# Attention scores over 64 of TensorE's 128 rows: even row tiles in the lower half, odd ones in the upper

## The chip, the cores and the metric

The kernel runs on one core of one Trainium2 chip. The metric is device time in microseconds (us) of one execution. Besides TensorE (PE in the profile; its weight loads are PEld) the core has VectorE (DVE), ScalarE (ACT), GpSimd (POOL) and the DMA queues issued from SyncE (SP) and POOL. They run side by side and meet at semaphores.

## The reference

Attention over 4 batches and 8 heads of 768 positions and 64 numbers each, with a window of 96 positions back and 8 global positions, and then two mixtures of experts over the 3072 rows:

```python
def _attn_ref(q, k, v, n_global, n_local):
    scores = scale * np.matmul(q, k.transpose(0, 1, 3, 2))
    keep = is_global | is_local                 # j < 8, or 0 <= i - j < 96
    scores = scores + bias[None, :, :, :]       # -slope[h] * distance
    scores = np.where(keep, scores, -1000000000.0)
    a = softmax(scores)
    return np.matmul(a, v)

def reference(**kwargs):
    x = _attn_ref(...)                          # to rows of 512
    x = _moe_ref(x=x, ...)                      # 8 experts, 512 -> 1024 -> 512
    return _moe2_ref(x=x, ...)                  # the same with a bias by modality
```

## The kernel before

A setup block builds constants, starts the first loads and works out on DVE whether the window fits the banded form (`banded`). In the banded form `banded_attention` runs; `general_attention` is compiled beside it and not executed with these inputs. After attention come routing and the two mixtures (`stages`), which the change leaves alone but for the tiles in which the second gate's weights wait.

Attention is cut into **slots**, one for each head of each batch (32, and two to run out). All engines go through the same slots in the order written out in their function `slot`. In slot h, TensorE does, in this order:

- `score(h, 0)` and `score(h, 1)`. A score takes one row tile of 128 queries against 256 keys (row tile 0: 128 keys) into one of three PSUM banks, `t.ps_s[:, n % 3]`. It waits until DVE has taken the score three before.
- one unit of `transpose_qk` for the next pair of heads (three 128x128 transposes into half 0 or 1 of `t.ps_qk`), then `weigh_v` on row tiles 2 to 5 of head h-2 (16 matmuls of 65 columns)
- `transpose_p(h-1, 0)`, `score` 2 and 3, the next unit of `transpose_qk`, `transpose_p(h-1, 1)`, `weigh_v` on row tiles 0 and 1 of head h-1
- in even slots `logits` (6 x 2 matmuls of 8 columns), then `score` 4 and 5, and `transpose_p(h-1, 2)`; in odd slots `transpose_x` before and after it, for the pair of heads finished last.

Every f32 matmul is two instructions in the trace, so a pair of scores is "x4".

A pair of heads has four units: units 0 and 1 are turned in the even slot and carry q, units 2 and 3 in the odd slot and carry k. A unit of q holds three row tiles of both heads: after the transpose head 2p lies in partitions 0 to 63 and head 2p+1 in 64 to 127. ACT's `move_qk` copies it to `t.qT` with two instructions of 64 partitions each (lines 512 and 513), one for each head. In `t.qT` each head has all 128 partitions, the half that is not its own being zero (lines 138 and 139 write these zeros once). So the matmul contracts over 128 rows, and the keys of the other head are multiplied by zero. The keys are copied with all partitions at once: the 8 global keys (line 517) and three blocks of 128 (line 519).

On ACT the unit moved in a slot stands behind exponentials 1 and 3 of that slot, and `move_x` (line 527), two copies of the finished pair's transpose, behind the sixth in odd slots. TensorE waits for `qk_moved` before the first score of an even slot and before each unit of `transpose_x`; it waits for `xT_moved` before it turns units 0 and 1.

DVE takes each score (`bias`, line 425), copies the turned probabilities (`move_pT`, line 434), and `finish`es a head (lines 440 to 446).

POOL stores zeros to the padding rows of `x2` (called mixed in the trace) out of the zero half of `t.qT` (line 198) and loads and splits the first expert's weights through the ring `t.stage`, all beside attention.

Of the kernel before, what the change touches and what calls it, by code (L numbers as in the profile page):

```python
# [12 lines left out]
P = 128  # L13
B, H, S, DH = 4, 8, 768, 64
NQ = S // P
# [62 lines left out]
def setup_block(nc, t, s, q, k, v, n_global, n_local, w_gate, w_gate2, mod_bias):  # L78

    with nc.Block() as block:  # L80
# [45 lines left out]
        def _(dve):  # L126
# [11 lines left out]
            dve.memset(t.qT[DH:P, 0, :, :], 0.0)  # L138
            dve.memset(t.qT[0:DH, 1, :, :], 0.0)

# [18 lines left out]
def banded_attention(t, s, q, k, v, x1, x2, w1, w2, modality_id):  # L159

    NS = H * NQ
    QKU = 4 * H // 2
# [28 lines left out]
    def gpsimd(pool):  # L191

        pool.dma_start(t.modi[:, :, :], modality_id.bitcast(I32)
                       .rearrange("(i p w) -> p i w", p=P, w=2)).then_inc(s.modality_loaded, 16)
        pool.wait_ge(s.rows_loaded, 1)

        for j in range(NT + 1, MAXT + 1):
            pool.dma_start(x2[j * P:(j + 1) * P, :].rearrange("(p r) n -> p (r n)", r=2),
                           t.qT[DH:P, 0, :, :].rearrange("p j n -> p (j n)")[:, 0:2 * D])\
                .then_inc(s.x2_cleared, 16)  # L200
# [15 lines left out]
        pool.wait_ge(s.x2_cleared, 16 * (MAXT - NT))  # L216

    def sync(sp):
        flag = sp.value_load(t.banded[0:1, 0:1], min_val=0, max_val=1)
        with sp.If_eq(sp.to_reg(flag), 1):  # L220
            def load(b, p):

                sp.wait_ge(s.qk_turned, QKU * b - QKU + 4 * p + 4)
# [29 lines left out]
    def tensor(pe):  # L253
        flag = pe.value_load(t.banded[0:1, 0:1], min_val=0, max_val=1)
        with pe.If_eq(pe.to_reg(flag), 1):
            def transpose_qk(b, p, first, units):
                for u in units:
                    if u == 0:
                        pe.wait_ge(s.qk_loaded[p % NPR], 64 * b + (p // NPR + 1) * 64)
                    src = t.q if u < 2 else t.k  # L260

                    pe.wait_ge(s.qk_moved, QKU * b + 4 * p + u + 1)
# [30 lines left out]
            def score(b, h, i):  # L293
# [5 lines left out]
                lhs = t.qT[:, h % 2, p % 2, i * P:(i + 1) * P]  # L299
# [3 lines left out]
                last = pe.matmul(t.ps_s[:, n % 3, c:c + w], lhs, t.kT[:, p % 2, k0:k0 + w],  # L303
# [24 lines left out]
            def slot(b, h, has_h, has_g, has_f, first=False, last=False):  # L328
                g, f = h - 1, h - 2
                if first and h == 0:  # L330
                    transpose_qk(b, 0, first, range(4))
                pair, units = next_units(h, has_h, last)
                if has_h and not (first and h == 0):
                    if h % 2 == 0:

                        pe.wait_ge(s.qk_moved, QKU * b + 2 + 4 * (h // 2) + 4)
# [8 lines left out]
                if first and h == 0:  # L345
                    pe.wait_ge(s.qk_moved, QKU * b + 2 + 4)
# [21 lines left out]
                turned = QKU * b + (4 * min(h // 2 + 2, NPR if last else NPR + 1) if has_h else 0)  # L368
# [131 lines left out]
    def scalar(act):  # L500
        flag = act.value_load(t.banded[0:1, 0:1], min_val=0, max_val=1)
        with act.If_eq(act.to_reg(flag), 1):
# [3 lines left out]

            def move_qk(b, p, units):
                for u in units:
                    act.wait_ge(s.qk_turned, QKU * b + 4 * p + u + 1)
                    cols = slice((u % 2) * 3 * P, (u % 2 + 1) * 3 * P)  # L510
                    if u < 2:
                        act.activation(t.qT[0:DH, 0, p % 2, cols], t.ps_qk[0:DH, u % 2, 0:3 * P], ACT.Copy)
                        last = act.activation(t.qT[DH:P, 1, p % 2, cols], t.ps_qk[DH:P, u % 2, 0:3 * P], ACT.Copy)
                    else:
                        blocks = t.kT[:, p % 2, :].rearrange("p (j w) -> p j w", w=OWN)
                        if u == 2:
                            act.activation(blocks[:, :, 0:GK],
                                           t.ps_qk[:, 0, 0:GK].unsqueeze(1).to_broadcast([P, NQ, GK]), ACT.Copy)
                        last = act.activation(blocks[:, 3 * (u % 2):3 * (u % 2) + 3, GK:OWN],
                                              t.ps_qk[:, u % 2, 0:3 * P].rearrange("p (j n) -> p j n", n=P),  # L520
                                              ACT.Copy)
# [8 lines left out]
            def slot(b, h, has_h, has_g, has_f, first=False, last=False):  # L530
                if first and h == 0:
                    move_qk(b, 0, range(4))
# [27 lines left out]
def general_attention(t, s, q, k, v, x1):  # L560
# [3 lines left out]
    def sync(sp):  # L564
        flag = sp.value_load(t.banded[0:1, 0:1], min_val=0, max_val=1)
        with sp.If_eq(sp.to_reg(flag), 0):
# [3 lines left out]
            with sp.Fori(0, B) as b:  # L570
                with sp.Fori(0, H) as h:
                    n = b * H + h
                    sp.wait_ge(s.g_head, n + 1)
                    for dst, src in ((t.q[:, :, 0:DH], qf), (t.k[:, :, 0:DH], kf), (t.v[:, :, 0, 0:DH], vf)):
# [13 lines left out]
    def tensor(pe):  # L588
        flag = pe.value_load(t.banded[0:1, 0:1], min_val=0, max_val=1)
        with pe.If_eq(pe.to_reg(flag), 0):  # L590
            with pe.Fori(0, B * H) as n:
                pe.wait_ge(s.g_loaded, 48 * n + 48)
                for u in range(4):
                    src = t.q if u < 2 else t.k
                    pe.wait_ge(s.g_moved, 4 * n + u + 1)
                    hold(pe, s.passed_pe)
                    for j in range(3):
                        last = pe.transpose(t.ps_qk[0:DH, 0, j * P:(j + 1) * P],
                                            src[:, 3 * (u % 2) + j, 0:DH], t.ident[:, :])
                    last.then_inc(s.g_turned, 1)  # L600
                pe.wait_ge(s.g_moved, 4 * n + 5)
                for i in range(NQ):

                    pe.wait_ge(s.g_done, NQ * n + i + 1)
                    for c, w in ((0, 512), (512, 256)):
                        last = pe.matmul(t.ps_s[:, c // 512, 0:w], t.qT[0:DH, 0, 0, i * P:(i + 1) * P],
                                         t.kT[0:DH, 0, c:c + w], start=True, stop=True)
# [23 lines left out]
    def scalar(act):  # L631
        flag = act.value_load(t.banded[0:1, 0:1], min_val=0, max_val=1)
        with act.If_eq(act.to_reg(flag), 0):
            act.sem_inc(s.g_moved, 1)
            with act.Fori(0, B * H) as n:
                for u in range(4):
                    act.wait_ge(s.g_turned, 4 * n + u + 1)
                    dst = t.qT[0:DH, 0, 0, :] if u < 2 else t.kT[0:DH, 0, :]
# [308 lines left out]
def load_gate2(sp, t, s, w_gate2):  # L947

    sp.wait_ge(s.attended, 1)
    for dst, d0, d1 in ((t.q, 0, DQ), (t.k, DQ, D)):  # L950
        sp.dma_start(dst[:, :, :].rearrange("p i n -> p (i n)")[:, 0:(d1 - d0) * E],
# [4 lines left out]
def spread_gate2(act, t, s):  # L956

    act.wait_ge(s.wg2_loaded, 32)
    for src, d0, d1 in ((t.q, 0, DQ), (t.k, DQ, D)):
        act.activation(t.wg2[:, :, d0:d1], src[:, :, :].rearrange("p i n -> p (i n)")[:, 0:(d1 - d0) * E]  # L960
# [456 lines left out]
def program(nc, q, k, v, n_global, n_local, moe_w_gate, moe_w1, moe_w2, modality_id, moe2_w_gate,  # L1417
# [6 lines left out]
    with keep:  # L1424
# [45 lines left out]
        with ExitStack() as a:  # L1470

            sb("beside_first_weights", [P, 2, WBUF], F32R, a)
            t.q = sb("q_rows", [P, NQ, D], F32, a)
            t.k = sb("k_rows", [P, NQ, D], F32, a)
            t.v = sb("v_rows", [P, NQ, H, VW], F32, a)
# [3 lines left out]
            t.qT = sb("qT", [P, 2, 2, S], F32, a)  # L1479
            t.kT = sb("kT", [P, 2, NQ * OWN], F32, a)  # L1480
# [63 lines left out]
        s.x2_cleared = sem("x2_cleared")  # L1544
# [129 lines left out]
```

## Time and profile before

| | us |
|---|---|
| median of 3 runs | 1046.38 (1045.7 to 1046.77) |
| the profiled execution's own time | 1046.11 |
| its span | 1044.2 |
| attention in steady state | about 24 to 272 in the span |
| routing between attention and the experts | about 272 to 303 |
| the experts | about 303 to 1044 |
| mean granted TensorE clock | 0.961 of 2.4 GHz |

The times in a timeline are counted from the span's start. A row "x4" merges four instructions; its length runs from the first start to the last end. Matmuls are pipelined, so the next row's start lies before the end of the one ahead. "Idle before" names what ended the wait; "issue" means that the profile shows nothing that was waited for.

### The profile page before, as it was taken

The numbers are of one execution on the slowest core, as the hardware profiler recorded it, in microseconds if no ns is written. First come the engines' busy times: TensorE is split into PE (matmuls) and PEld (weight loads), VectorE is DVE, ScalarE is ACT, GpSimd is POOL, SyncE is SP. The second block draws the span as 40 slices with busy tenths as digits, with TensorE's granted clock in tenths as the row PEclk, the third lists the DMA queues.
The fourth block names the chain that finished last, engine by engine and source line by source line (L and its number), as shares of the span: only waits on it lengthen the run. The fifth ranks groups of instructions, "written<-read, shape, count | busy, mean of one in ns | idle before, by whom it ended". The sixth has DMA issues, their size and how long they took to land.

```text
span 1044.2 us, 18844 instructions
## 1 busy us (share of the span) xinstructions
PE 965.2 (92%) x5357; PEld 818.0 (78%) x5358; DVE 619.0 (59%) x1644; ACT 391.5 (37%) x722; POOL 185.8 (18%) x259
## 2 busy tenths in 40 slices
PE   4999999999659999999999999639999999999994
PEld 3899999999547888888888888437888888888883
DVE  5766666666479888897896969694222225222231
ACT  3665565564162425333352433033222225222230
POOL 2273000000021111231221211012112112121110
PEclk9999999999669999999999999859999999999997
DMA  9898754720333333352452515014111115111110
GB/s 149 205 279 169 147 124 97 144 60 26 102 112 125 128 121 121 135 188 81 169 174 67 200 51 201 20 47 166 40 40 40 50 41 193 40 40 50 40 40 9
DMA packets 138521, 110.42 MB, mean 106 GB/s; under 512 B 101887, under 2 KB 114223, under 8 KB 138352
## 3 DMA queue, kind: packets, MB, share of 16 engines
q1 hardware_dynamic: 127440, 74.51, 27.0%
q0 software_dynamic: 11040, 35.42, 10.2%
q8 instruction: 19, 0.31, 0.1%
q14 instruction: 22, 0.18, 0.1%
HBM read 87.36 MB, written 23.33 MB: 106 GB/s over the span
## 4 chain that ended last, share of the span: by engine, by line
PE 88%; DVE 6%; issue 2%; DMA 1%; SPq 1%; DVEq 0%; ACT 0%; POOL 0%; POOLq 0%
PE PS L1135 29%; PE PS L1115 28%; PE PS L325 8%; PE PS L303 8%; PE PS L1123 4%; PE PS L313 4%; PE PS L1104 2%; PE PS L268 2%; PE PS L289 2%; PE PS L280 1%; DVE W L1243 1%; DMA k_rows<-in_k_dram 0%; SPq L56 0%; DMA xin<-attended,gather_rows 0%; DVE products L1254 0%
## 5 line engine op out<-in xcount | busy, mean ns | idle before, releaser
L1135 PE MATMUL PS<-W,hT_high 128*128 (+1 forms) x880 | 283.5, 404 | 3.9 <-DVE hT_low L1301 3.9
L1115 PE MATMUL PS<-W,xT_high 128*128 (+1 forms) x880 | 279.6, 399 | 6.2 <-DVE xT_low L1234 6.2
L1135 PEld LDWEIGHTS PS<-W,hT_high 128*128 128x128 f32 x880 | 162.9, 190 | 39.9 <-issue 4.3
L1115 PEld LDWEIGHTS PS<-W,xT_high 128*128 128x128 f32 x880 | 163.0, 190 | 38.8 <-DVE xT_low L1234 4.4
L1135 PE MATMUL PS<-W,hT_low 128*128 (+1 forms) x440 | 175.4, 399 | 0.0
L1115 PE MATMUL PS<-W,xT_low 128*128 (+1 forms) x440 | 173.6, 394 | 0.0
L1215 ACT ACTIVATE hT_high<-PS 128x512 fp32r<-128x512 f32 x110 | 59.8, 596 | 284.7 <-PE PS L1123 284.7
L1254 DVE CUSTOM_DVE_ANT_0 products<-y,gate_columns 128x512 f32<-128x512 f32 x236 | 148.8, 687 | 0.3 <-DVE logits_of_rows L1254 0.3
L1211 ACT ACTIVATE h<-PS 128x512 f32<-128x512 f32 x110 | 65.6, 597 | 176.3 <-PE PS L1115 176.3
L1262 DVE TENSOR_SCALAR y<-PS,gate 128x512 f32<-128x512 f32 x57 | 42.8, 751 | 146.4 <-PE PS L1135 142.9
L538 ACT ACTIVATE pbuf<-biased_scores,nmax 128x256 f32<-128x256 f32 (+1 forms) x192 | 87.3, 488 | 107.0 <-DVE nmax L425 105.5
L1234 DVE TENSOR_TENSOR xT_low<-PS,xT_high 128x512 fp32r<-128x512 f32 x57 | 39.3, 690 | 138.2 <-ACT xT_high L1197 136.9
L1135 PEld LDWEIGHTS PS<-W,hT_low 128*128 128x128 f32 x440 | 83.6, 190 | 20.0
L1115 PEld LDWEIGHTS PS<-W,xT_low 128*128 128x128 f32 x440 | 83.5, 190 | 18.5
L303 PE MATMUL PS<-kT,qT 128*128 128x256 f32 (+1 forms) x384 | 96.5, 374 | 1.3 <-DVE nmax L425 0.6
L1243 DVE TENSOR_TENSOR W<-stage,W 128x1024 f32 (+1 forms) x80 | 92.6, 1220 | 1.0 <-ACT W L1205 1.0
L425 DVE CUSTOM_DVE_ANT_0 biased_scores<-PS,bias 128x256 f32<-128x256 f32 (+1 forms) x192 | 72.9, 399 | 23.7 <-issue 12.3
L1205 ACT ACTIVATE W<-stage 128x1024 f32 (+1 forms) x80 | 78.5, 1060 | 6.5 <-DVE na_i L861 5.5
L1042 POOL DMA_INDIRECT xin<-attended,gather_rows x30 | 32.1, 1070 | 231.8 <-DVE na_i L861 207.5
L1301 DVE TENSOR_TENSOR hT_low<-PS,hT_high 128x512 fp32r<-128x512 f32 x110 | 70.8, 685 | 3.4
L325 PE MATMUL PS<-v_rows,pT 128*128 128x65 f32 x384 | 68.5, 274 | 2.1 <-DVE pT L434 2.0
L303 PEld LDWEIGHTS PS<-kT,qT 128*128 128x128 f32 x384 | 61.8, 194 | 5.9 <-DVE nmax L425 1.5
(226 smaller groups left out, 1084.5 us busy)
## 6 DMA issues: line engine op xcount, KB each, us to landing
stage<-in_moe_w_dram SPq DMA_DIRECT2D x80, 512.0 KB, 4.7
mixed<-y POOLq DMA_DIRECT2D x30, 256.0 KB, 2.3
q_rows<-in_q_dram SPq DMA_DIRECT2D x32, 192.0 KB, 3.7
k_rows<-in_k_dram SPq DMA_DIRECT2D x32, 192.0 KB, 4.1
v_rows<-in_v_dram SPq DMA_DIRECT2D x32, 192.0 KB
attended<-x_rows SPq DMA_DIRECT2D x16, 384.0 KB, 3.3
v_before<-in_v_dram SPq DMA_DIRECT2D x32, 150.0 KB
stage<-in_moe_w_dram POOLq DMA_DIRECT2D x8, 512.0 KB, 9.3
```

Source lines behind the costliest of these rows:

```text
L303: last = pe.matmul(t.ps_s[:, n % 3, c:c + w], lhs, t.kT[:, p % 2, k0:k0 + w], start=True, stop=True)
L325: last = pe.matmul(out, lhs, rhs, start=n == 0, stop=n == len(terms) - 1)
L425: dve.tensor_tensor_reduce(out=t.sb[:, n % 3, 0:w], in0=t.ps_s[:, n % 3, c:c + w], in1=t.bias[:, h, o:o + w], scale=-SCALE, scalar=3.0e38, ...
L538: act.activation(t.pbuf[:, h % 2, i, c:c + w], t.sb[:, n % 3, 0:w], ACT.Exp, bias=t.nmax[:, h % 2, i:i + 1], scale=-1.0).then_inc(s.exped, 1)
L1115: last = pe.matmul(t.PS[:, f, :], lhs[:, c, :], t.W[:, bass.ds(w + part, 512)], start=c == 0 and n == 0, stop=c == KD - 1 and n == 2)
L1135: last = pe.matmul(t.PS[:, 2, :], lhs[:, c, :], t.W[:, bass.ds(off + (c * D + part), D)], start=c == 0 and n == 0, stop=c == KF - 1 and n ...
L1205: act.activation(t.W[:, bass.ds(other + k * WCH, WCH)], t.stage[:, k % RING, :], ACT.Copy).then_inc(m.w_hi, 1)
L1211: act.activation(t.h[:, f * 512:(f + 1) * 512], t.PS[:, f, :], ACT.Relu).then_inc(st.h_ready, 1)
L1215: act.activation(t.hTh[:, 4 * f:4 * f + 4, :].rearrange("p c n -> p (c n)"), t.PS[:, 3 + f, :], ACT.Copy).then_inc(st.h_high, 1)
L1243: dve.tensor_tensor(t.W[:, bass.ds(other + (k * WCH + WBUF), WCH)], t.stage[:, k % RING, :], t.W[:, bass.ds(other + k * WCH, WCH)].bitcast ...
L1254: dve.tensor_tensor_reduce(out=t.products[:, e % 2, :], in0=t.y[:, :], in1=t.wg2[:, e, :], scale=1.0, scalar=0.0, op0=ALU.mult, op1=ALU.ad ...
L1301: dve.tensor_tensor(t.hTl[:, 4 * f:4 * f + 4, :].rearrange("p c n -> p (c n)"), t.PS[:, 3 + f, :], t.hTh[:, 4 * f:4 * f + 4, :].rearrange( ...
```

## The change

- The scores contract over 64 rows. Row tile i of a head takes half i % 2 of the partitions: `lhs` and the keys are `t.qT[half, ...]` and `t.kT[half, ...]`, with half 0 the partitions 0 to 63 and half 1 the rest. Two scores that follow each other thus use different halves.
- q is loaded by head: `t.q` is `[P, H, NQ, DH]` instead of `[P, NQ, H*DH]`. Unit u of q (0 or 1) is now one head of the pair, and each of its three transposes takes two row tiles of that head, the even one into the lower half, the odd one into the upper. `move_qk` copies it with one instruction of 128 partitions instead of two of 64.
- Each head needs its keys in both halves. `t.kT` has a second copy with the halves exchanged, written by two more copies of 64 partitions for each copy of 128: units 2 and 3 take 3 x 3 copies in all instead of 3.
- The zeros in `t.qT` and the two memsets that wrote them are gone. The padding rows of `x2` are cleared from `t.stage[:, 0]`, which POOL fills with zeros first, with 128 rows of 2 KB for each DMA instead of 64 of 4 KB. POOL waits for these 8 DMAs before its first weight load instead of at its end.

The order of instructions on TensorE, DVE and SP is as before. The core of the diff:

```diff
-            sp.dma_start(dst[:, :, h * DH:(h + 1) * DH] if which == "qk" else dst[:, :, h, 0:DH],
+            sp.dma_start(t.q[:, h, :, :] if dst is t.q else t.k[:, :, h * DH:(h + 1) * DH] if which == "qk" else
+                         dst[:, :, h, 0:DH],
...
-            dve.memset(t.qT[DH:P, 0, :, :], 0.0)
-            dve.memset(t.qT[0:DH, 1, :, :], 0.0)
...
+        pool.memset(t.stage[:, 0, :], 0.0).then_inc(s.blank, 1)
         pool.wait_ge(s.rows_loaded, 1)
-
+        pool.wait_ge(s.blank, 1)
         for j in range(NT + 1, MAXT + 1):
-            pool.dma_start(x2[j * P:(j + 1) * P, :].rearrange("(p r) n -> p (r n)", r=2),
-                           t.qT[DH:P, 0, :, :].rearrange("p j n -> p (j n)")[:, 0:2 * D])\
-                .then_inc(s.x2_cleared, 16)
+            pool.dma_start(x2[j * P:(j + 1) * P, :], t.stage[:, 0, 0:D]).then_inc(s.x2_cleared, 16)
+        pool.wait_ge(s.x2_cleared, 16 * (MAXT - NT))
...
-                        i = 3 * (u % 2) + j
-                        last = pe.transpose(t.ps_qk[:, u % 2, j * P:(j + 1) * P],
-                                            src[:, i, p % NPR * P:(p % NPR + 1) * P], t.ident[:, :])
+                        rows = t.q[:, 2 * (p % NPR) + u, 2 * j:2 * j + 2, :].rearrange("p i d -> p (i d)") if u < 2 \
+                            else t.k[:, 3 * (u - 2) + j, p % NPR * P:(p % NPR + 1) * P]
+                        last = pe.transpose(t.ps_qk[:, u % 2, j * P:(j + 1) * P], rows, t.ident[:, :])
...
-                lhs = t.qT[:, h % 2, p % 2, i * P:(i + 1) * P]
+                half = slice(i % 2 * DH, (i % 2 + 1) * DH)
+                lhs = t.qT[half, p % 2, h % 2, i // 2 * P:(i // 2 + 1) * P]
...
-                last = pe.matmul(t.ps_s[:, n % 3, c:c + w], lhs, t.kT[:, p % 2, k0:k0 + w],
+                last = pe.matmul(t.ps_s[:, n % 3, c:c + w], lhs, t.kT[half, p % 2, (h + i) % 2, k0:k0 + w],
...
+            low, high = slice(0, DH), slice(DH, P)
+            KEYS = [(0, slice(0, P), slice(0, P)), (1, low, high), (1, high, low)]
...
                     if u < 2:
-                        act.activation(t.qT[0:DH, 0, p % 2, cols], t.ps_qk[0:DH, u % 2, 0:3 * P], ACT.Copy)
-                        last = act.activation(t.qT[DH:P, 1, p % 2, cols], t.ps_qk[DH:P, u % 2, 0:3 * P], ACT.Copy)
+                        last = act.activation(t.qT[:, p % 2, u, :], t.ps_qk[:, u, 0:3 * P], ACT.Copy)
...
+                            for a, into, out in KEYS:
+                                act.activation(keys(p, a, into)[:, :, 0:GK], ...)
+                        for a, into, out in KEYS:
+                            last = act.activation(keys(p, a, into)[:, 3 * (u % 2):3 * (u % 2) + 3, GK:OWN],
+                                                  t.ps_qk[out, u % 2, 0:3 * P].rearrange("p (j n) -> p j n", n=P),
+                                                  ACT.Copy)
```

ACT, an odd slot of the kernel before (pbuf is the exponential's output, kT the keys, x_pairT the output of `move_x`):

```order
L538 ACTIVATE pbuf<-biased_scores,nmax 128x128
L538 ACTIVATE pbuf<-biased_scores,nmax 128x256
L517 ACTIVATE kT<-PS 128x6x8
L519 ACTIVATE kT<-PS 128x3x128
L538 ACTIVATE pbuf<-biased_scores,nmax 128x256 x2
L519 ACTIVATE kT<-PS 128x3x128
L538 ACTIVATE pbuf<-biased_scores,nmax 128x256 x2
L527 ACTIVATE x_pairT<-PS 128x384 x2
```

The same slot of the kernel with the change:

```order
L541 ACTIVATE pbuf<-biased_scores,nmax 128x128
L541 ACTIVATE pbuf<-biased_scores,nmax 128x256
L519 ACTIVATE kT<-PS 128x6x8
L519 ACTIVATE kT<-PS 64x6x8 x2
L522 ACTIVATE kT<-PS 128x3x128
L522 ACTIVATE kT<-PS 64x3x128 x2
L541 ACTIVATE pbuf<-biased_scores,nmax 128x256 x2
L522 ACTIVATE kT<-PS 128x3x128
L522 ACTIVATE kT<-PS 64x3x128 x2
L541 ACTIVATE pbuf<-biased_scores,nmax 128x256 x2
L530 ACTIVATE x_pairT<-PS 128x384 x2
```

Six copies were added ahead of the last two exponentials and of `move_x`. POOL, from the start of attention, before:

```order
L193 DMA modi<-in_moe_modality_id_dram 128x24x2
L198 DMA mixed<-qT 64x1024 x8
L204 DMA stage<-in_moe_w_dram 128x1024 x4
L211 CAST W<-stage 128x1024
L213 TENSOR_TENSOR W<-stage,W 128x1024
```

And with the change:

```order
L192 DMA modi<-in_moe_modality_id_dram 128x24x2
L194 MEMSET stage 128x1024
L198 DMA mixed<-stage 128x512 x8
L203 DMA stage<-in_moe_w_dram 128x1024 x4
L210 CAST W<-stage 128x1024
L212 TENSOR_TENSOR W<-stage,W 128x1024
```

A memset stands ahead of the clearing DMAs, and these read `stage`.

## Rows read from the trace of the kernel before

**Rows 1.** The page: span, busy time of TensorE, the chain that ended last.
```profile
span 1044.2 us, 18844 instructions
...
PE 965.2 (92%) x5357; PEld 818.0 (78%) x5358; DVE 619.0 (59%) x1644; ACT 391.5 (37%) x722; POOL 185.8 (18%) x259
...
PE PS L1135 29%; PE PS L1115 28%; PE PS L325 8%; PE PS L303 8%; PE PS L1123 4%; PE PS L313 4%; PE PS L1104 2%; PE PS L268 2%; PE PS L289 2%; PE PS L280 1%; DVE W L1243 1%; DMA k_rows<-in_k_dram 0%; SPq L56 0%; DMA xin<-attended,gather_rows 0%; DVE products L1254 0%
```

**Rows 2.** Busy us of each engine in stretches: PE, PEld, DVE, ACT, POOL, clock, DMA.
```profile
24.00:272.00 248.00, 244.80 (x1866) 225.66 (x1865) 157.90 (x587) 136.03 (x321) 36.35 (x32) 0.99 0.61 134
```

**Rows 3.** Timeline of PE, 154 to 170 us: start, length, line, shape, count.
```profile
154.31 0.52 PE L268 MATMUL PS<-ident,q_rows 128*128 128x128 f32 x3
...
158.48 0.56 PE L325 MATMUL PS<-v_rows,pT 128*128 128x65 f32 x4
...
160.41 1.11 PE L303 MATMUL PS<-kT,qT 128*128 128x256 f32 x4
161.35 0.49 PE L313 MATMUL PS<-ident,pbuf 128*128 128x128 f32 x3
161.68 0.82 PE L303 MATMUL PS<-kT,qT 128*128 128x128 f32 x4
162.34 0.49 PE L268 MATMUL PS<-ident,k_rows 128*128 128x128 f32 x3
162.67 0.43 PE L325 MATMUL PS<-v_rows,pT 128*128 128x65 f32 x2
...
164.50 0.61 PE L313 MATMUL PS<-ident,pbuf 128*128 128x128 f32 x4
164.94 1.03 PE L303 MATMUL PS<-kT,qT 128*128 128x256 f32 x4
165.80 0.49 PE L268 MATMUL PS<-ident,k_rows 128*128 128x128 f32 x3
...
168.76 0.49 PE L280 MATMUL PS<-ident,x_rows 128*128 128x128 f32 x3
169.09 0.82 PE L303 MATMUL PS<-kT,qT 128*128 128x128 f32 x4
169.94 0.52 PE L268 MATMUL PS<-ident,q_rows 128*128 128x128 f32 x3
```

**Rows 4.** Timeline of ACT, 163 to 170 us, an odd slot.
```profile
163.83 0.49 ACT L519 ACTIVATE kT<-PS 128x384 f32<-128x384 f32 x1
166.65 0.91 ACT L538 ACTIVATE pbuf<-biased_scores,nmax 128x256 f32<-128x256 f32 x2 [2.33 <-DVE nmax L425]
167.46 0.47 ACT L519 ACTIVATE kT<-PS 128x384 f32<-128x384 f32 x1
168.48 0.94 ACT L538 ACTIVATE pbuf<-biased_scores,nmax 128x256 f32<-128x256 f32 x2 [0.55 <-DVE nmax L425]
169.32 0.85 ACT L527 ACTIVATE x_pairT<-PS 128x384 f32<-128x384 f32 x2
...
170.97 0.47 ACT L512 ACTIVATE qT<-PS 64x384 f32<-64x384 f32 x1
```

**Rows 5.** PE's weight loads: one wait in the timeline, and waits by cause, 24 to 270 us.
```profile
169.91 0.31 PEld L268 LDWEIGHTS PS<-ident,q_rows 128*128 128x128 f32 x3 [0.40 <-issue]
...
PEld PS L268 <- issue: 4.4, 11, 0.4
PEld PS L268 <- ACT x_pairT L527: 0.7, 2, 0.3
```

**Rows 6.** Timeline of DVE at the copies ahead of the two parts of `weigh_v`.
```profile
157.51 0.68 DVE L434 COPY pT<-PS 128x512 f32<-128x512 f32 x1
...
162.05 0.55 DVE L434 COPY pT<-PS 128x384 f32<-128x384 f32 x1
```

**Rows 7.** Groups by line and shape, 20 to 290 us: busy us, mean ns of one.
```profile
L303 PEld LDWEIGHTS PS<-kT,qT 128*128 128x128 f32 x380 | 60.8, 193 | 4.9 <-DVE nmax L425 1.5
```

**Rows 8.** Timeline of DVE in the setup block.
```profile
3.31 1.34 DVE L139 MEMSET qT<- 64x1536 f32 x1 [0.36 <-issue]
4.73 0.17 DVE L143 CAST parf<-par 128x2 f32<-128x2 int32 x1
```

**Rows 9.** Timeline of POOL: its clearing DMAs and the last split of the first weights.
```profile
39.68 4.23 POOL L198 DMA_DIRECT2D mixed<-qT  x8 [29.93 <-SPq L242]
...
85.36 2.36 POOL L213 TENSOR_TENSOR W<-stage,W 128x1024 fp32r<-128x1024 f32 x1
```

More of the change, by code:

```diff
@@ L330, in slot @@
                 if first and h == 0:
-                    transpose_qk(b, 0, first, range(4))
+                    transpose_qk(b, 0, first, range(QKP))
                 pair, units = next_units(h, has_h, last)
@@ L367, in slot @@
                     score(b, h, 5)
-                turned = QKU * b + (4 * min(h // 2 + 2, NPR if last else NPR + 1) if has_h else 0)
+                turned = QKU * b + (QKP * min(h // 2 + 2, NPR if last else NPR + 1) if has_h else 0)
                 if h % 2 == 1 and has_f:
@@ L505, in scalar, with keys @@
             act.sem_inc(s.xT_moved, 2)
+            low, high = slice(0, DH), slice(DH, P)
+            KEYS = [(0, slice(0, P), slice(0, P)), (1, low, high), (1, high, low)]
+            def keys(p, a, part):
+                return t.kT[part, p % 2, a, :].rearrange("p (j w) -> p j w", w=OWN)
             def move_qk(b, p, units):
                 for u in units:
-                    act.wait_ge(s.qk_turned, QKU * b + 4 * p + u + 1)
-                    cols = slice((u % 2) * 3 * P, (u % 2 + 1) * 3 * P)
+                    act.wait_ge(s.qk_turned, QKU * b + QKP * p + u + 1)
                     if u < 2:
-                        act.activation(t.qT[0:DH, 0, p % 2, cols], t.ps_qk[0:DH, u % 2, 0:3 * P], ACT.Copy)
-                        last = act.activation(t.qT[DH:P, 1, p % 2, cols], t.ps_qk[DH:P, u % 2, 0:3 * P], ACT.Copy)
+                        last = act.activation(t.qT[:, p % 2, u, :], t.ps_qk[:, u, 0:3 * P], ACT.Copy)
                     else:
-                        blocks = t.kT[:, p % 2, :].rearrange("p (j w) -> p j w", w=OWN)
                         if u == 2:
[L517 to L521, printed above, removed]
+                            for a, into, out in KEYS:
+                                act.activation(keys(p, a, into)[:, :, 0:GK], t.ps_qk[out, 0, 0:GK].unsqueeze(1)
+                                               .to_broadcast([out.stop - out.start, NQ, GK]), ACT.Copy)
+                        for a, into, out in KEYS:
+                            last = act.activation(keys(p, a, into)[:, 3 * (u % 2):3 * (u % 2) + 3, GK:OWN],
+                                                  t.ps_qk[out, u % 2, 0:3 * P].rearrange("p (j n) -> p j n", n=P),
+                                                  ACT.Copy)
                     last.then_inc(s.qk_moved, 1)
@@ L531, in slot @@
                 if first and h == 0:
-                    move_qk(b, 0, range(4))
+                    move_qk(b, 0, range(QKP))
                 pair, units = next_units(h, has_h, last)
@@ L573, in sync @@
                     sp.wait_ge(s.g_head, n + 1)
-                    for dst, src in ((t.q[:, :, 0:DH], qf), (t.k[:, :, 0:DH], kf), (t.v[:, :, 0, 0:DH], vf)):
+                    for dst, src in ((t.q[:, 0, :, :], qf), (t.k[:, :, 0:DH], kf), (t.v[:, :, 0, 0:DH], vf)):
                         sp.dma_start(dst, src[bass.ds(n, 1), :, :, :]
@@ L605, in tensor @@
                     for c, w in ((0, 512), (512, 256)):
-                        last = pe.matmul(t.ps_s[:, c // 512, 0:w], t.qT[0:DH, 0, 0, i * P:(i + 1) * P],
-                                         t.kT[0:DH, 0, c:c + w], start=True, stop=True)
+                        last = pe.matmul(t.ps_s[:, c // 512, 0:w], t.qTf[0:DH, i * P:(i + 1) * P],
+                                         t.kTf[0:DH, c:c + w], start=True, stop=True)
                     last.then_inc(s.g_scored, 1)
@@ L949, in load_gate2 @@
     sp.wait_ge(s.attended, 1)
-    for dst, d0, d1 in ((t.q, 0, DQ), (t.k, DQ, D)):
-        sp.dma_start(dst[:, :, :].rearrange("p i n -> p (i n)")[:, 0:(d1 - d0) * E],
+    for dst, d0, d1 in ((t.qf, 0, DQ), (t.kf, DQ, D)):
+        sp.dma_start(dst[:, 0:(d1 - d0) * E],
                      w_gate2[d0:d1, :].rearrange("(a d) e -> a (d e)", a=1)
```

34 lines of the change are left out of this document (19 added, 15 removed).

## The prediction

> **What bounds the kernel now.** I read the page first: TensorE is busy 92% of the span, and the chain that ended last is mostly TensorE's, with 8% on line 303, the scores [rows 1]. The change touches attention alone, so the next view is busy time by stretch: from 24 to 272 us TensorE is busy 244.8 of 248 us at a granted clock of 0.99, while ACT has 136 and DVE 158 [rows 2]. What attention gains or loses moves all that follows. But busy shares hide how the engines hand over, so I took one pair of slots and followed it in the timelines.
>
> The pair runs from one unit 0 of `transpose_qk` to the next: 154.31 to 169.94 on TensorE, 15.6 us [rows 3], 16 times in the program. I cut it where another engine stands right behind TensorE:
>
> - **A**, from unit 0 (154.31) to `weigh_v` of row tiles 0 and 1 (158.48). DVE's copy that this needs ends at 157.51 + 0.68 = 158.19 [rows 6]. TensorE is late by 0.29 us; about 0.1 of it is the way of a semaphore, as between ACT and TensorE below. Slack on DVE: 0.19 us.
> - **B**, from there to `weigh_v` of row tiles 2 to 5 in the odd slot (162.67). DVE's copy ends at 162.05 + 0.55 = 162.60 [rows 6, 3]. Slack: none. That copy stands behind DVE's steps on scores 4 and 5, which follow the first score's end, so two scores that end sooner together don't bring it forward.
> - **C**, those 16 matmuls, 162.67 to 164.50.
> - **D**, from there to the next unit 0. The row before it, scores 0 and 1, starts at 169.09 and streams 0.66 us, as the same row does at 161.68 (162.34 follows). TensorE would be ready at 169.75 and starts at 169.94 [rows 3]. Its weight load was late by 0.40 us, at 169.91. Eleven of these waits have no name in the profile and two more have that of `move_x` [rows 5]. The timeline of ACT names the others: the first `move_x` starts at 169.32, ends at 169.8, and the load comes 0.1 behind [rows 4]. Unit 0 waits for just that semaphore. So here ACT is the bound, by 0.19 us.
>
> All three engines are nearly level. That decides what a saving on one of them is worth.
>
> **The change, part by part.**
>
> *Overlap of scores.* Four score matmuls of 256 columns go in 165.80 - 164.94 = 0.86 us, 0.215 each; with a first tile of 128 keys four take 0.66, so a short one 0.115 [rows 3]. The order in a pair is A-high, A-low, B-high, B-low. B lies in the other half of the rows and in another PSUM bank. As issue is in order, B-high can run at the earliest beside A-low, and B-low behind B-high: three steps instead of four. That saves 0.215 for each of two pairs and 0.11 for the pair with the short tile: 0.54 us a slot, 1.08 a pair of slots, 17.3 us in 32 slots. It is the upper end. The lower is nothing, if halves don't overlap. The trace has no 64-row matmul. I take the overlap as real.
>
> *Switching between 128 and 64 rows.* All around the scores still uses 128 rows ("128*128" in every row [rows 3]). Each pair of scores is an island: three a slot, in and out, 6 switches a slot, 12 a pair of slots, 190 in all (two islands touch at the start). The trace has no switch. Lower bound: nothing. The nearest row for an array that must run empty is a matmul's length beyond its streaming: the four scores at 164.94 are listed as 1.03 us and give way after 0.86, so 0.17 us [rows 3]. If the next weights can't be loaded meanwhile either, the whole load of 0.19 [rows 7] comes on top: 0.36. I take 0.17, because the load behind the wait at 169.91 cost only 0.03 before the matmul started [rows 5, 3].
>
> The Trainium skill, "TensorEngine Tiling (Array Packing)", Key Properties, says that changing the tiling mode drains TensorE, and gives no price. By that rule the switches cost something and the lower bound of nothing would be out; no run here shows it yet. The same skill, "TensorE: Matmul & The Clock Gate", Part 3, has matmuls in different row groups starting some 4 ns apart, which is the overlap taken above.
>
> *Copies on ACT.* For q one copy of 0.47 replaces two, at a place with idle time ahead. For k each block copy becomes three, since a 64-partition copy takes 0.47 as a 128-partition one does [rows 4]. Unit 2 (163.83) grows by some 1.2 us and has 2.33 us of idle behind it: hidden. Unit 3 starts at 167.46, right behind an exponential, and ends 0.96 later than now, at 168.90. The next exponential now starts at 168.48. Thus exponentials 4 and 5, and `move_x` behind them, move by 0.42 us, and unit 0 of the next pair with them. That is D at +0.42 instead of +0 if TensorE gains there. Two waits on the way, scores 0 at 169.09 and the second `transpose_x` at 168.76, need unit 3 moved; the latter then comes 0.3 to 0.4 late, but inside the same 0.42.
>
> *Setup.* Two memsets of 1.34 us go. The next DVE step starts 0.08 behind the second [rows 8]. The two loads that it needs were issued shortly before, so it may start sooner by anything from 0 to 1.3 us; I take 0. If the cover is gone it is a gain of up to 1.3.
>
> *POOL and DMA.* The clearing DMAs start at 39.68 and the last split of weights is at 85.36, some 200 us before the experts need them [rows 9, 2]. A memset, one landing time and 2 KB rows vanish in that. The loads of q move the same 256-byte pieces. Both at nothing.
>
> **The sum**, for each pair of slots, with 0.17 a switch. A: 2 switches +0.34, overlap -0.215: +0.125. B: 4 switches +0.68, overlap -0.325: +0.355. C: 0. D: 6 switches +1.02, overlap -0.54, and the present wait of 0.19 fills up: +0.29 for TensorE, but ACT asks +0.42, so +0.42. Together +0.90, times 16 = +14.4 us. On the profiled execution's own time, 1046.1 (span 1044.2, 1.9 around it; median of the runs 1046.4), that is **1060.5 us**.
>
> **Rivals.**
>
> 1. *No price for a switch; ACT's copies decide.* With overlap: A at most -0.19 (DVE's slack), B 0, D +0.42: +0.23, some 3.6 us over the 15 or 16 pairs. Without overlap +0.42 each, 6 us. Taken together 1051. For it: TensorE's tile is only a mask as far as the trace shows. Against: nothing measured.
> 2. *A dearer switch, or no overlap.* With 0.265 a switch, halfway between 0.17 and 0.36: A +0.315, B +0.735, D +0.86, 1.91 x 16 = 30.6 us, 1076.7. With 0.17 and no overlap, so that the change doesn't do what it says: +0.34, +0.68, +0.83 = 1.85, 29.6 us, 1075.7. The extreme, 0.36 with overlap, is 48.8 us, 1095.
> 3. *Faster: the overlap passes through.* If switches are free, the score pairs end 1.08 us sooner for each pair of slots, and if DVE then takes its steps sooner as well, because it is only following TensorE, B and A give their full gain and only D's 0.42 is lost: -0.66 x 16 = -10.6, 1035.5; with D hidden too, 1028.8. It decides below 0.05 us a switch (12 switches against 0.66). Against it: the ends of DVE's copies in A and B, 0.1 to 0.3 ahead of TensorE.
>
> **How the numbers follow.** The forecast (0.17 a switch, 1053 to 1068) has 0.38, rival 1 0.28, rival 2 0.26, rival 3 0.08. A measurement of this kernel tells 0.2%, 2.1 us, from no change. Faster by more is rival 3: 0.08. Within it lies the lower edge of rival 1, with the gain in setup: 0.06. Slower: 0.86. The range goes from 1047, which takes in nearly all of rival 1, to 1088, where rival 2 has most of itself: outside are rival 3 (0.08), the extreme of rival 2 (0.08) and a rest of rival 1 (0.03). The two large unknowns, a switch and the overlap, make it this wide.
>
> **What would show it.** In the timeline of the changed kernel, the start of the row behind four scores against their own start: 0.86 means neither overlap nor price, 0.65 overlap, and more than 0.9 a price; likewise from the row ahead to the scores. The scores' rows should read 64*128. `move_x` should begin 0.4 later behind its slot's exponential 3, and unit 0 behind it. The pair should last 16.5 us. I am wrong if the pair is under 15.6, and the price is wrong if the pair is near 15.9 or over 17.2. The stretch of the experts should be unchanged.

## The result, and the profile after

The changed kernel takes 1074.4 us (median of 4 runs, 1070.3 to 1077.9) against 1046.6 before (4 runs, 1045.7 to 1047.4): a ratio of 1.026, 95% interval 1.023 to 1.030. It is slower by 27.8 us. The forecast was 1060.5, range 1047 to 1088.

The profiled execution took 1077.9 us with a span of 1076.2. First the page of the kernel after: busy time, and TensorE's busy share and granted clock in 40 slices of 27 us. They answer to [rows 1].

```profile
span 1076.2 us, 18908 instructions
...
PE 991.4 (92%) x5357; PEld 809.6 (75%) x5358; DVE 615.3 (57%) x1642; ACT 411.5 (38%) x786; POOL 187.9 (17%) x260
...
PE   4999999999957999999999999927999999999995
...
PEclk9998779898867999999999999967999999999998
```

The same clock line of the kernel before:

```profile
PEclk9999999999669999999999999859999999999997
```

Before, attention (slices 1 to 10) runs at the full clock, 2.4 GHz. After, it has slices of 7 and 8 tenths: TensorE's granted clock fell to its lower level, 1.2 GHz, five times inside steady attention and once more in the last slots. The forecast has no word on that. Busy time by stretch shows it more closely (columns as in [rows 2]; the first number is the length of the stretch):

```profile
80.00:88.00 8.00, 8.00 (x63) 6.69 (x63) 4.57 (x19) 3.32 (x9) 6.76 (x5) 1.00 1.09 197
88.00:98.00 10.00, 10.00 (x45) 8.42 (x44) 3.73 (x14) 5.40 (x14) 0.00 (x0) 0.50 0.40 83
...
108.00:122.00 14.00, 14.00 (x61) 11.17 (x61) 5.89 (x23) 7.81 (x19) 0.00 (x0) 0.52 0.53 111
122.00:146.00 24.00, 23.50 (x185) 19.12 (x182) 13.98 (x54) 12.85 (x32) 0.00 (x0) 1.00 0.47 96
146.00:160.00 14.00, 14.00 (x61) 10.99 (x59) 5.61 (x21) 7.68 (x19) 0.00 (x0) 0.51 0.57 116
```

63 matmuls in 8 us at 1.00, 45 in 10 us at 0.50. A busy share can't tell: it is full in both.

Now the pair of slots, from one unit 0 to the next. At the full clock it usually lasts 16.08 us (7 pairs between 16.0 and 16.4), against 15.62. Five pairs with a stretch at 0.5 in them last 18.8 to 21.6. Here is one pair at full clock, 160.06 to 176.26, a little longer than usual at 16.20 us, and of the next, of 16.08 us, the rows at which its parts are cut. It is the timeline of PE after and answers to [rows 3]:

```profile
160.06 0.55 PE L266 MATMUL PS<-ident,q_rows 128*128 128x128 f32 x3
...
162.19 0.61 PE L311 MATMUL PS<-ident,pbuf 128*128 128x128 f32 x4
162.72 0.70 PE L301 MATMUL PS<-kT,qT 64*128 64x256 f32 x4
163.36 0.55 PE L266 MATMUL PS<-ident,q_rows 128*128 128x128 f32 x3
163.74 0.60 PE L311 MATMUL PS<-ident,pbuf 128*128 128x128 f32 x4
164.18 0.57 PE L323 MATMUL PS<-v_rows,pT 128*128 128x65 f32 x4
...
167.30 0.95 PE L301 MATMUL PS<-kT,qT 64*128 64x128 f32 x4
168.18 0.55 PE L266 MATMUL PS<-ident,k_rows 128*128 128x128 f32 x3
168.57 0.33 PE L323 MATMUL PS<-v_rows,pT 128*128 128x65 f32 x2
...
174.87 0.55 PE L277 MATMUL PS<-ident,x_rows 128*128 128x128 f32 x3 [0.33 <-ACT kT L522]
175.34 0.70 PE L301 MATMUL PS<-kT,qT 64*128 64x128 f32 x4
176.26 0.52 PE L266 MATMUL PS<-ident,q_rows 128*128 128x128 f32 x3 [0.22 <-ACT x_pairT L530]
...
180.34 0.56 PE L323 MATMUL PS<-v_rows,pT 128*128 128x65 f32 x4
...
184.72 0.33 PE L323 MATMUL PS<-v_rows,pT 128*128 128x65 f32 x2
...
192.34 0.52 PE L266 MATMUL PS<-ident,q_rows 128*128 128x128 f32 x3 [0.22 <-ACT x_pairT L530]
```

**The overlap is whole.** The four scores at 162.72 give way after 0.64 us, which looks like the three steps of 0.215 that I had written down. But it is two steps and a price. Cut to 162.7 to 162.9, the view shows two matmuls whose first start and last end lie 0.49 apart. The same cut of the kernel before, around 165.1, gives 0.60 for two:

```profile
162.72 0.49 PE L301 MATMUL PS<-kT,qT 64*128 64x256 f32 x2
```

```profile
164.94 0.60 PE L303 MATMUL PS<-kT,qT 128*128 128x256 f32 x2
```

The view of line 301 in the same four (shortest, median and longest in ns, first and last start) gives the lengths of one:

```profile
L301 PE MATMUL PS<-kT,qT x4: 376/428/480, 162.7 to 163.0; 64*128 64x256 f32 x4
```

The first two take 480 ns each and 0.49 together, so they start together; the other two start together at 163.0, 0.3 behind. Which is which can be told from the trace's records: the two at 162.72 each wait for DVE and give no signal, which makes them A-high and B-high, and the two at 163.04 each give the signal that ends a score, which makes them A-low and B-low. B-high starts ahead of A-low, which stands before it in the program. So there are two steps of 0.215, 0.43 in all, not three. What is above 0.43 belongs to the switches.

**A switch costs 0.17, as taken.** Around the scores at 162.72, the four transposes ahead give way after 0.53 instead of 0.44 (+0.09), the scores after 0.64 instead of 0.43 (+0.21), the transposes behind after 0.38 instead of 0.33 (+0.05). That is 0.35 us an island, 0.175 a switch. The weight loads show where it goes. PEld after, with idle time ahead of the first load in the new form:

```profile
162.72 0.30 PEld L301 LDWEIGHTS PS<-kT,qT 64*128 64x128 f32 x4 [0.17 <-issue]
163.35 0.31 PEld L266 LDWEIGHTS PS<-ident,q_rows 128*128 128x128 f32 x3 [0.33 <-issue]
```

In the kernel before the next weights are loaded while a matmul streams; here the load and the first matmul in the new form start together, once the stream in the old form has run out. A kernel with small 64-row matmuls ahead of 128-row scores, further on, agrees with this price without any overlap. By the Trainium skill, "TensorEngine Tiling (Array Packing)", Key Properties, a change of tiling mode drains the engine: the trace agrees, at 0.175 us.

**ACT** in the same odd slot, answering to [rows 4]:

```profile
172.54 0.91 ACT L541 ACTIVATE pbuf<-biased_scores,nmax 128x256 f32<-128x256 f32 x2 [1.10 <-DVE nmax L423]
173.35 1.46 ACT L522 ACTIVATE kT<-PS 128x384 f32<-128x384 f32 x3
174.84 0.91 ACT L541 ACTIVATE pbuf<-biased_scores,nmax 128x256 f32<-128x256 f32 x2
175.65 0.85 ACT L530 ACTIVATE x_pairT<-PS 128x384 f32<-128x384 f32 x2
```

Unit 3 takes three copies, 1.46 us; no idle is left ahead of the exponential behind it, and `move_x` starts 2.30 us behind unit 3 instead of 1.86: +0.44.

**Where the time went.** The experts' first transposes start here (line of `xin`: count, lengths in ns, first and last start), before and after:

```profile
L1104 PE MATMUL PS<-ident,xin x228: 270/272/477, 299.0 to 1016.9; 128*128 128x128 f32 x114
```

```profile
L1107 PE MATMUL PS<-ident,xin x228: 270/272/474, 330.6 to 1050.5; 128*128 128x128 f32 x114
```

All of the difference, 31.6 us of this execution, lies ahead of that point; the experts last 745.6 us against 745.2. Of the 31.6, 21.3 are the five pairs with a stretch at 0.5 (4.7, 5.5, 5.5, 2.8, 2.8 over 16.08), 2.8 are in two early pairs (20.06 to 47.86, 27.8 us against 25.0; the clock rises at 29.9 instead of 23.2), 5.7 are the other 0.47 for each of the twelve pairs behind them, and 1.8 are in the last slots, where the clock fell once more.

### The profile page after: what moved, and what is told of

It is laid out like the page before. It is cut to its first block, busy times and chain, and to the rows that moved or that the text cites. A ratio compares the mean times of both kernels' runs of the same rounds, so it can differ in the third digit from the quotient of the medians.

```text
span 1076.2 us, 18908 instructions
## 1 busy us (share of the span) xinstructions
PE 991.4 (92%) x5357; PEld 809.6 (75%) x5358; DVE 615.3 (57%) x1642; ACT 411.5 (38%) x786; POOL 187.9 (17%) x260
## 3 DMA queue, kind: packets, MB, share of 16 engines
q1 hardware_dynamic: 127440, 74.51, 25.9%
## 4 chain that ended last, share of the span: by engine, by line
PE 84%; DVE 7%; issue 3%; ACT 3%; SPq 1%; DVEq 0%; DMA 0%; POOL 0%; ACTq 0%; POOLq 0%
PE PS L1138 28%; PE PS L1118 27%; PE PS L323 8%; PE PS L301 5%; PE PS L1126 4%; PE PS L311 3%; PE PS L266 3%; PE PS L1107 2%; PE PS L286 2%; ACT kT L522 1%; ACT pbuf L541 1%; DVE W L1246 1%; ACT x_pairT L530 0%; DMA k_rows<-in_k_dram 0%; SPq L56 0%
## 5 line engine op out<-in xcount | busy, mean ns | idle before, releaser
L423 DVE CUSTOM_DVE_ANT_0 biased_scores<-PS,bias 128x256 f32<-128x256 f32 (+1 forms) x192 | 70.6, 399 | 41.1 <-PE PS L301 27.0
L301 PE MATMUL PS<-kT,qT 64*128 64x256 f32 (+1 forms) x384 | 80.4, 456 | 3.7 <-ACT kT L522 3.5
L323 PE MATMUL PS<-v_rows,pT 128*128 128x65 f32 x384 | 74.1, 292 | 2.0 <-DVE pT L432 1.9
L323 PE MATMUL PS<-v_before,pT 128*128 128x65 f32 x320 | 69.4, 302 | 0.0
```

What stands on the lines that cost most here:

```text
L301: last = pe.matmul(t.ps_s[:, n % 3, c:c + w], lhs, t.kT[half, p % 2, (h + i) % 2, k0:k0 + w], start=True, stop=True)
L323: last = pe.matmul(out, lhs, rhs, start=n == 0, stop=n == len(terms) - 1)
L423: dve.tensor_tensor_reduce(out=t.sb[:, n % 3, 0:w], in0=t.ps_s[:, n % 3, c:c + w], in1=t.bias[:, h, o:o + w], scale=-SCALE, scalar=3.0e38, ...
```

## The experiments

Two things wanted a cause: the 0.46 us for each pair at full clock, and the falls of the clock. The theories at the start: (1) the switches bring the clock down; (A) the waits for ScalarE's added copies do; later (1b) 64-row work does, (C) the share of gaps does, (D) it is how many rows work.

**One part alone: 64 rows, no overlap, no second keys.** From the kernel before:

```diff
-                lhs = t.qT[:, h % 2, p % 2, i * P:(i + 1) * P]
+                half = slice(h % 2 * DH, (h % 2 + 1) * DH)
+                lhs = t.qT[half, h % 2, p % 2, i * P:(i + 1) * P]
...
-                last = pe.matmul(t.ps_s[:, n % 3, c:c + w], lhs, t.kT[:, p % 2, k0:k0 + w],
+                last = pe.matmul(t.ps_s[:, n % 3, c:c + w], lhs, t.kT[half, p % 2, k0:k0 + w],
```

> The kernel before with one edit: each score contracts over the 64 rows of its own head (both scores of a pair in the same half, so no overlap); zeros, keys and all copies on ScalarE as before. Theory 1 (a switch costs some 0.07 us of TensorE time, read from the changed kernel's trace, and the load that waits at each switch lowers TensorE's activity so that its clock falls to 0.5 now and then): a pair of slots at full clock lasts 15.6 - 0.19 + 12 x 0.07 = 16.3 us, and there are stretches at clock 0.5 within attention; 1060 to 1080 us. Rival A (the clock falls because TensorE waits for ScalarE's added copies): no stretch at 0.5 before attention ends, 1046 + 16 x 0.65 = 1056 us. Rival B (0.17 a switch, as predicted): a pair lasts 17.5 us, 1076 us or more.

Measured: 1300.8 us (1257.8 to 1303.4, 4 runs). That is far beyond every expectation; even the quickest run is 1.20 times the kernel before. In the profiled execution, of 1301.7 us, a pair lasts 32.27 us. The timeline of PE and the stretch:

```profile
104.97 2.07 PE L304 MATMUL PS<-kT,qT 64*128 64x256 f32 x4
106.97 0.90 PE L268 MATMUL PS<-ident,q_rows 128*128 128x128 f32 x3
```

```profile
100.00:132.00 32.00, 32.00 (x121) 26.12 (x120) 10.65 (x37) 9.41 (x22) 0.00 (x0) 1.00 0.30 60
```

```profile
L268 PE MATMUL PS<-ident,q_rows x96: 417/418/476, 9.1 to 462.4; 128*128 128x128 f32 x96
```

The last row counts all transposes of q in the program: the shortest takes 417 ns. In the kernel before the median is 273. So all of attention ran at 1.2 GHz in this execution; the clock never rose. The column of the granted clock reads 1.00 in that stretch and is wrong: it is filled from recorded changes, and the first on record is at 560.8 us, past attention. The lengths decide. There are no added copies on ACT here, so a low clock doesn't need them, against (A). The run can't price a switch at the full clock, and what made the quickest run 44 us shorter isn't shown: its trace wasn't kept.

**The change without the second keys.** From the changed kernel:

```diff
-            KEYS = [(0, slice(0, P), slice(0, P)), (1, low, high), (1, high, low)]
+            KEYS = [(0, slice(0, P), slice(0, P))]
...
-t.kT[half, p % 2, (h + i) % 2, k0:k0 + w]
+t.kT[half, p % 2, 0, k0:k0 + w]
```

> The changed kernel without the second copy of the keys (all scores read the first copy, so odd row tiles meet the other head's keys: that part of the scores is not the reference's). 64 rows and alternating halves stay. Theory 1 (ScalarE's copies make the full-clock pair 16.08 us, the switches the clock): the full-clock pair falls to 15.4 to 15.7 us, stretches at 0.5 stay; 1060 to 1070 us. Rival A (the waits for the copies bring the clock down): no stretch at 0.5 in attention, under 1046 us.

Measured: 1100.9 us (4 runs, 1086.5 to 1113.0). Pairs at full clock last 15.67 to 16.07 us, the quickest 0.4 shorter than in the changed kernel, and near the 15.62 of the kernel before: the copies are what the full-clock pair had too much. But in the profiled execution, the slowest of the four, the clock fell in seven of fourteen pairs. All four runs are slower than all four of the changed kernel (1070.3 to 1077.9), with less waiting. The waits for the added copies are not what brings the clock down there.

**The copies alone.** From the kernel before, with 128-row scores that read the first copy; the second is read by nobody:

```diff
+            KEYS = [(0, slice(0, P), slice(0, P)), (1, low, high), (1, high, low)]
...
+                        for a, into, out in KEYS:
+                            last = act.activation(keys(p, a, into)[:, 3 * (u % 2):3 * (u % 2) + 3, GK:OWN], ...)
```

> The kernel before with 128-row scores, and on ScalarE the six added copies of keys for each pair of heads, into a second tile that nobody reads. Theory 1: unit 3 ends 0.96 us later and move_x 0.42 later, so a pair lasts 15.62 + 0.42 = 16.04 us, no stretch at 0.5 in attention: 1046 + 15 x 0.42 = 1052.5 us. Rival A (waits for these copies bring the clock down): stretches at 0.5, 1065 us or more.

Measured: 1056.1 us (4 runs, 1055.9 to 1057.5), ratio 1.0095 (1.0072 to 1.0118). Unit 0 follows unit 0 here:

```profile
132.10 0.52 PE L268 MATMUL PS<-ident,q_rows 128*128 128x128 f32 x3 [0.20 <-ACT x_pairT L534]
...
148.15 0.49 PE L268 MATMUL PS<-ident,q_rows 128*128 128x128 f32 x3
```

16.05 us, and 15.96 to 16.17 in eleven of twelve pairs, against 16.04 expected. Within steady attention the clock stays up. One stretch of 6.8 us at 0.5 lies at the start, from 34.6 us; ahead of it TensorE had waited 2.02 us for ACT's copies of keys (31.0 to 33.06). So a fall can follow one long wait; none follows the waits of 0.20 us in this kernel's steady attention. That wait and the fall are most of what the start lost (6.7 us up to the fourth unit 0, 51.81 instead of 45.10), and the start is the rest of the difference. So part D of the sum, +0.42, is shown: the added copies alone cost a pair 0.43, nearly all that a full-clock pair of the changed kernel loses. Overlap and switches together add little to it, 0.05 by the quickest pair without the second keys (15.67 against 15.62), some of which the wait for `move_x` may hide.

**Switches alone.** From the kernel before, a small 64-row matmul ahead of each pair of scores:

```diff
+                if i % 2 == 0:
+                    pe.matmul(t.ps_s[:, n % 3, c:c + 8], t.qT[0:DH, h % 2, p % 2, i * P:(i + 1) * P],
+                              t.kT[0:DH, p % 2, k0:k0 + 8], start=True, stop=True)
```

> The kernel before with 128-row scores and one added matmul of 64 rows and 8 columns (two instructions) ahead of each pair of scores, so the same 12 switches for each pair of slots, but all real work on 128 rows. Theory 1a (switching itself, with its empty array and late loads, lowers the activity): stretches at clock 0.5 in attention; a pair at full clock 15.43 + 6 x (2 x 0.07 + two small matmuls of 0.1) = 17.5 us at most; 1065 to 1090 us. Theory 1b (it is the 64-row work that counts as less activity): no stretch at 0.5, 1065 to 1076 us from the added time alone.

Measured: 1089.0 us (4 runs, 1083.7 to 1091.3), ratio 1.040. Unit 0 to unit 0:

```profile
127.18 0.49 PE L268 MATMUL PS<-ident,q_rows 128*128 128x128 f32 x3
...
129.78 0.39 PE L304 MATMUL PS<-kT,qT 64*128 64x8 f32 x2
130.09 1.13 PE L306 MATMUL PS<-kT,qT 128*128 128x256 f32 x4
131.06 0.49 PE L268 MATMUL PS<-ident,q_rows 128*128 128x128 f32 x3
...
145.39 0.49 PE L268 MATMUL PS<-ident,q_rows 128*128 128x128 f32 x3
```

18.21 us, so (18.21 - 15.43) / 6 = 0.46 for two switches and two small matmuls; with 0.35 for the switches it leaves 0.11 for the matmuls, which nothing measures apart. I had set 0.07 for a switch, and the expectation's own upper end of 17.5 was passed: 0.17 fits and 0.07 doesn't. The four scores at 130.09, right behind a switch and without any overlap, give way after 0.97 instead of 0.86: the switch back alone puts 0.11 on them. Past one stretch of 3.4 us at 61.4 the clock stays at 1.00 for all of attention. The switches are the same 12 as in the first experiment. There the clock never rises, here it stays up in steady attention. What differs, beside the small matmuls, is whether the scores work on 64 rows or on 128. Half of these 128 rows multiply the zeros in `t.qT`, so it isn't the useful rows that count.

**Twice the scores in the changed kernel.**

```diff
+                for _ in range(2):
                     last = pe.matmul(t.ps_s[:, n % 3, c:c + w], lhs, t.kT[half, p % 2, (h + i) % 2, k0:k0 + w],
```

> The changed kernel with every score issued twice (same result): the same number of switches, twice the 64-row work. Theory 1b (64-row work is what lets the clock fall, since a kernel with the same switches and 128-row work kept it): more stretches at 0.5 than in the changed kernel, perhaps no rise at all; more than 1130 us. Rival C (the gaps at the switches do it, and longer islands dilute them): fewer stretches at 0.5; a pair of slots at full clock 16.1 + 2.6 = 18.7 us, 1046 + 16 x 3.1 = 1096 us.

Measured: 1083.7 us (4 runs, 1083.1 to 1084.6), ratio 1.036. The clock doesn't fall in attention before its last steps, at 307.7 us:

```profile
80.00:300.00 220.00, 219.80 (x1764) 183.28 (x1764) 123.79 (x456) 122.88 (x300) 7.56 (x5) 1.00 0.42 89
```

192 scores more cost 9 us more than the changed kernel's median. Pairs last 17.9 instead of 18.7, since the added scores overlap too: two added steps of 0.215 in each of four islands, and less in the two with a short tile. (1b) in its plain form falls: this is more 64-row work, and the clock is up. (C) would explain it. Or, (D), two halves at work together are as good as 128 rows, and longer islands of that kind make up for the gaps.

**Twice the scores without overlap** tells these apart: the first experiment's kernel with the same loop. The switches and the number of matmuls are those of the experiment above, but only one half works at a time (and there are no second keys).

> The first experiment's kernel (64-row scores, both of a pair in the same half, no second keys) with every score issued twice. Beside the changed kernel with its scores twice it differs in that the two halves never work together. Theory D (what keeps the clock up is how many rows work, so two halves together count as a full array and one half alone does not): clock 0.5 through most of attention, 1330 us or more. Rival C (only the gaps at the switches count, and longer islands dilute them): the clock rises and stays as it did there; a pair of slots 15.43 + 2.1 + 4.8 = 22.3 us, 1046 + 16 x 6.7 = 1153 us.

Measured: 1431 us (two runs, 1413 and 1449; the profiled one is the longer). Pairs of 41.67 us, and again no transpose of q under 417 ns:

```profile
L268 PE MATMUL PS<-ident,q_rows x96: 417/421/478, 9.0 to 594.1; 128*128 128x128 f32 x96
```

The other run's mean granted clock, 0.771 over 1411 us, comes by an estimate to 646 us at the lower level, so it was low for most of attention there too. (C) expected 1153 and is out as the only cause; (D) stands.

**Twice the switches, 128-row scores.** The small matmul ahead of every score:

> The kernel before with 128-row scores and a matmul of 64 rows and 8 columns ahead of every score: 24 switches for each pair of slots instead of 12. Price of a switch: with the same 0.46 us for each island of two switches and two small matmuls, a pair lasts 15.43 + 12 x 0.46 = 21.0 us, 1046 + 16 x 5.5 = 1134 us. Theory 1b (64-row work lowers the clock): the clock stays at 1.0 within attention past the start. Rival C (gaps do it): stretches at 0.5, well over 1150 us.

Measured: 1263 us (4 runs, 1243 to 1275), some 1.2 times the kernel before. A pair at full clock lasts 21.28 us (62.35 to 83.63), against 21.0 expected. But every pair behind it has a stretch at 0.5 and lasts 27.5 to 30.7:

```profile
93.00:106.00 13.00, 13.00 (x51) 10.93 (x49) 4.11 (x16) 3.41 (x8) 0.00 (x0) 0.50 0.33 64
107.00:120.00 13.00, 13.00 (x88) 11.04 (x89) 5.81 (x21) 5.54 (x13) 0.00 (x0) 1.00 0.31 62
```

So twice the switches, and the gaps that they make, bring the clock down with all real work on 128 rows. This fits theory (D) if it is widened: what the clock answers to is how much of the array works over time, where one half is less than two and a gap is nothing. All runs here agree with that, but it is an inference: none of them changes the rows or the gaps alone within the changed kernel, so how much each has in its falls isn't shown.

**The wait for `move_x`.** Both kernels with the first of its two copies ahead of the last exponential:

```diff
                         move_qk(b, pair, units[i // 2:i // 2 + 1])
-                if h % 2 == 1 and has_f:
-                    move_x(b, h // 2 - 1)
+                    if i == 4 and h % 2 == 1 and has_f:
+                        move_x(b, h // 2 - 1, [0])
+                if h % 2 == 1 and has_f:
+                    move_x(b, h // 2 - 1, [1] if has_h else [0, 1])
```

> The kernel before with the first of the two copies of move_x placed between exponentials 5 and 6 of an odd slot instead of behind both. If ScalarE bounds part D by 0.19 us as read from the timelines, a pair goes from 15.62 to 15.43 us and the time falls by 14 x 0.19 = 2.7 us, to 1043.8 us. Rival: another wait takes its place, 1046.4 us.

Measured on the kernel before: 1043.9 us (12 runs) against 1046.6 (17 runs), ratio 0.9979 (0.9967 to 0.9992). The pair went from 15.62 to 15.40 and unit 0 follows the scores after 0.66 us, with no wait:

```profile
167.93 0.82 PE L303 MATMUL PS<-kT,qT 128*128 128x128 f32 x4
168.59 0.49 PE L268 MATMUL PS<-ident,q_rows 128*128 128x128 f32 x3
```

This is quicker than both kernels, by 2.7 us, as expected; the interval leaves 1 out.

> The changed kernel with the same edit. The copy starts 0.4 us sooner, so the full-clock pair goes from 16.08 to some 15.7 us, as without the second keys; with the stretches at 0.5 as in the changed kernel 1060 to 1075 us. Rival (the second transpose_x, which waits for unit 3, is the bound): 16.08 stays.

Measured on the changed kernel: 1082.2 us (4 runs, 1074.1 to 1088.4). The full-clock pair went from 16.08 to 15.82, less than I said, since the second `transpose_x` still waits for unit 3. And in the profiled execution the clock fell in four pairs, for 13.7 us each time, 54.6 us in all, against 51.2 in the five pairs of the changed kernel. The gain at full clock, some 4 us, didn't show in the median.

## Why the prediction came out as it did

**Direction and range held, but most of the amount came for a reason that wasn't in the forecast.** Forecast +14.4, measured +27.8. What the forecast reckoned with is worth some 7 us (16 pairs of 0.46), half of what it said; on that alone the time would have been near 1054, by estimate. The falls of the clock, which it didn't reckon with, made the rest. That the total lies in the range is in part luck.

1. *What bounds attention* was right: TensorE level with DVE and ACT, and ACT the bound in D by 0.19. Taking that wait away gave 0.22 a pair.
2. *The price of a switch*, 0.17 from the nearest row, was right: 0.175 in the timeline, and 0.46 for an island with its small matmuls in a kernel with nothing else changed. For a while, reading the first trace in haste, I gave it as 0.07, having counted the 0.64 us of a pair of scores as three steps. The experiment with small matmuls put that straight.
3. *The overlap* was mis-sized. The step that failed is "As issue is in order, B-high can run at the earliest beside A-low". Both high parts start together, so a full pair of scores saves 0.43, not 0.215. In the pair from 176.26 to 192.34, A came to 4.08 us against 4.17 (-0.09; forecast +0.125) and B to 4.38 against 4.19 (+0.19; forecast +0.355). The scores with the short tile gave less: at 167.30 the pair took 0.88 against 0.66. Its second score starts 0.26 behind the first, once DVE has taken the score three before.
4. *D*, +0.42 from ACT, was about right. With C, the usual pair has 7.62 (184.72 to 192.34) against 7.27, +0.35; the longer one before it has 7.69, +0.42. The copies alone gave 0.43 a pair.
5. The sum of these is +0.46 in the usual pair instead of +0.90, some 7 us over all. That is near rival 1 (0.23 to 0.42), though not for its reason: a switch isn't free, it is paid for by a larger overlap. The signs that the prediction named would have misled here. It took four scores that give way after 0.65 for overlap without a price, and a pair near 15.9 for a wrong price; 0.64 and 16.08 are near both, and yet the price was right. Both signs stood on three steps.
6. *The clock* was missing. None of the cases asked what 64 rows and gaps do to it; the grant of 0.99 in attention [rows 2] was taken as given. The five falls made 21.3 of the 31.6 us of the profiled execution, and with the later rise at the start and the fall in the last slots it is up to 25.9. I had no row for it, as the kernel before stays at the full clock in steady attention. It does leave it at 268.9 us, in the last slots, after 7 us in which TensorE was busy for 5.8: that was the row to ask.
7. Setup, POOL and the loads at nothing: right. The first unit 0 starts at 9.04 us against 9.01, the last split of weights at 84.57, long before the experts, and the experts are unchanged.

The four runs spread over 7.6 us, against 1.7 before. How much of that comes from more or fewer falls isn't shown, since one execution of each kernel was traced; the traces of the changed kernel and of its two variants have five, seven and four pairs with a fall.

## What to carry to other kernels

Half-height matmuls that alternate halves did run at the same time here, two for the price of one, where both were ready when the first was issued. But a pair has to buy back two switches of 0.17 us and whatever copies lay its operands out in both halves, and with 256 columns in f32 it just does (0.43 us saved, 0.35 paid). Where TensorE is the bound, ask of a change also what it does to the clock: less of the array at work, or more gaps, can cost more than all the steps that one can count. Here it was 21 us against 6 in twelve pairs.

## What the runs showed of the hardware

- A switch between 128*128 and 64*128 costs 0.175 us: the next weights are loaded only when the old stream has run out (0.17 and 0.33 us of idle on the load side).
- Two f32 matmuls of 64 rows in different halves and PSUM banks start within 0.01 us of each other (162.723 and 162.729), and the second starts ahead of a matmul that stands before it in the program and uses the first one's half (163.043).
- With every score issued twice and both halves at work, the clock stayed at 2.4 GHz through attention (24.4 to 307.7 us); with one half at a time, and the same switches and matmuls, it stayed at 1.2 GHz from 20 to 660 us, with TensorE busy for 640.0 of 640 us, and with every score issued once from 20 to 520 us, busy for 499.7 of 500. In the changed kernel itself, both halves at work kept it up only in part. The Trainium skill, "TensorE: Matmul & The Clock Gate", Part 1, ties the clock to how busy the engine has been; the traces agree only if busy isn't the profile's busy share, which is full in both; rows at work would fit.
- A granted clock of 1.00 can mean that no change was recorded. The length of a known row decides: 128-column transposes take 272 ns at 2.4 GHz and 417 at 1.2.
